# Three inputs of a linear-attention stage read head dimension first, and part of VectorE's work given to TensorE, ScalarE and GpSimd

## The reference

```
# 1. linear attention with a decaying state, per batch and head
for t in range(S):
    cur = einsum('d,e->de', u * k[t], v[t])
    y[t] = einsum('d,de->e', r[t], state + cur)
    state = w[t][:, None] * state + einsum('d,e->de', k[t], v[t])
# 2. mixture of 8 experts, top 2 by noisy gate, x = y as (3072, 384), F=1024
logits = x @ w_gate;  noisy = logits + log1p(exp(x @ w_noise)) * noise
out = sum over the two best e of weight_e * (relu(x @ w1[e]) @ w2[e])
# 3. feed forward, 2048 wide
h = out @ w_in;  result = (h - tanh(h)) @ w_out
```

## Time and profile before

| | |
|---|---|
| time, median of 3 runs | 1189.33 us (1189.25 to 1194.11) |
| the profiled execution | 1191.79 us, its span 1190.3 us |
| PE, DVE, ACT, POOL busy | 1104.0, 738.1, 567.3, 136.8 us |
| attention stage | from the start to about 227 us |
| experts, feed forward | to about 770 us, to the end |

### The profile page before, as it was taken

The page is one execution under the profiler, slowest core; times in us unless marked ns, Lnnn a source line. Parts: engine busy times, 40 slices in busy tenths (PEclk is TensorE's granted clock), DMA queues, the critical chain, the costliest instruction groups (busy, mean ns, idle before and its releaser), DMA issues.

```text
span 1190.3 us, 24896 instructions
## 1 busy us (share of the span) xinstructions
PE 1104.0 (93%) x8968; PEld 1053.2 (88%) x8968; DVE 738.1 (62%) x1036; ACT 567.3 (48%) x808; POOL 136.8 (11%) x188
## 2 busy tenths in 40 slices
PE   5888867789799999999999999999999999999998
PEld 4677756689799999999999999899999999999998
DVE  8999988638957777766677777643434333343433
ACT  5445433346347666666666666532332323333232
POOL 1000223212820000000000000221010101101010
PEclk9999889889999999999999999999999999999999
DMA  9664555556778888888888888511010101101010
GB/s 154 122 123 88 121 117 157 175 189 190 258 245 288 280 278 269 281 277 276 276 273 289 264 276 282 184 47 36 25 60 0 59 0 59 59 0 59 0 59 20
DMA packets 192751, 185.04 MB, mean 155 GB/s; under 512 B 98192, under 2 KB 160912, under 8 KB 192688
## 3 DMA queue, kind: packets, MB, share of 16 engines
q1 hardware_dynamic: 176208, 152.74, 44.8%
q0 software_dynamic: 6528, 20.06, 5.1%
q10 hardware_dynamic: 9952, 11.41, 2.8%
HBM read 156.85 MB, written 27.33 MB: 155 GB/s over the span
## 4 chain that ended last, share of the span: by engine, by line
PE 77%; DVE 13%; issue 5%; ACT 3%; SPq 1%; POOL 1%; DMA 1%; another core or an unknown queue 0%; DVEq 0%; ACTq 0%; POOLq 0%
PE ps L789 6%; PE ps L858 6%; PE ps L876 6%; PE ps L878 6%; PE ps L877 6%; PE ps L859 6%; PE ps L860 6%; PE ps L790 5%; PE ps L791 5%; PE ps L747 5%; PE ps L749 4%; PE ps L748 4%; PE ps L767 2%; PE ps L766 2%; PE ps L765 2%
## 5 line engine op out<-in xcount | busy, mean ns | idle before, releaser
L1590 DVE TENSOR_TENSOR w_lo<-w_raw,w_hi 128x1536 fp32r<-128x1536 f32 x140 | 244.3, 1755 | 93.3 <-ACT w_hi L909 88.1
L909 ACT ACTIVATE w_hi<-w_raw 128x1536 fp32r<-128x1536 f32 x140 | 206.5, 1488 | 24.8 <-ACT y_out L1101 12.3
L1590 DVE TENSOR_TENSOR gg<-ps,th 128x768 f32<-128x768 f32 x64 | 61.3, 957 | 168.3 <-ACT th L1148 168.3
L789 PE MATMUL ps<-w_hi,h_hi 128*128 128x384 f32 x440 | 151.0, 343 | 9.0 <-DVE h_lo L1674 8.3
L747 PE MATMUL ps<-xT_hi,w_hi 128*128 128x256 f32 x480 | 139.6, 291 | 10.9 <-issue 5.7
L791 PE MATMUL ps<-w_hi,h_lo 128*128 128x384 f32 x440 | 147.9, 336 | 0.0
L790 PE MATMUL ps<-w_lo,h_hi 128*128 128x384 f32 x440 | 147.9, 336 | 0.0
L1878 POOL DMA_INDIRECT yy<-yg,slot_g x54 | 54.2, 1004 | 751.3 <-DVE w_lo L1590 425.5
L749 PE MATMUL ps<-xT_hi,w_lo 128*128 128x256 f32 x480 | 137.2, 286 | 0.0
L748 PE MATMUL ps<-xT_lo,w_hi 128*128 128x256 f32 x480 | 137.1, 286 | 0.0
L876 PE MATMUL ps<-wout_hi,g_hi 128*128 128x384 f32 x384 | 130.4, 340 | 0.0
(11 more groups left out here) (266 smaller groups left out, 2088.1 us busy)
## 6 DMA issues: line engine op xcount, KB each, us to landing
w_raw<-in_moe_w SPq DMA_DIRECT2D x140, 768.0 KB
xt_in<-xg SPq DMA_DIRECT2D x20, 384.0 KB
yg<-y_out ACTq DMA_DIRECT2D x20, 384.0 KB
k_pad<-in_k SPq DMA_DIRECT2D x32, 144.0 KB, 3.9
v_nat<-in_v SPq DMA_DIRECT2D x32, 144.0 KB
out<-o_out SPq DMA_DIRECT2D x8, 576.0 KB
w_nat<-in_w SPq DMA_DIRECT2D x15, 288.0 KB, 3.3
r_pad<-in_r SPq DMA_DIRECT2D x30, 144.0 KB
```

The source lines that it names most:

```text
L789: pe.matmul(o, h_hi[:, f, cols], w2_hi[:, f, :], start=(f == 0), stop=False, skip_group_check=True)
L909: nc.scalar.activation(dst, src, ACT.Copy).then_inc(s, 1)
L1590: vec.tensor_tensor(dst, a, b, ALU.subtract).then_inc(s, 1)
```

## The change

The host hands over r, k and w transposed to head dimension first (`r_cols`, `k_cols`, `w_cols`), and v by pairs (`v_pairs`), beside the original arrays. They are loaded straight to where the scans and products read them, so `turn`, `straight`, `spread_in` and their buffers are gone. The cleared gaps between 48 and 64 partitions are now set by whole-buffer clears (`wz` by VectorE, `klin`, `rlin` by GpSimd). `wz` has two buffers. The range check is a ReLU with a sum along the row on ScalarE, once for each side of the range; VectorE only tests 8 sums to a batch. GpSimd makes `kr`. TensorE adds the bonus rows `bv` to the result in PSUM with two products with the identity, and ScalarE copies the result out (`tokens`). `betas` writes to the KV bank instead of A0.

```diff
@@ sync @@
+            def load_cols(e, dst, src, landed, n, h):
+                e.dma_start(dst[s][h * HB:h * HB + D, :], src[n // HP, 2 * (n % HP) + h]).then_inc(landed[s], 16)
 def next_w(n):
-                    sp.wait_ge(spread, n - 1)
-                    sp.wait_ge(w_squared, n - 1)
+                    sp.wait_ge(scanned, 2 * (n - 2) + 2)
+                    sp.wait_ge(w_checked, 2 * (n - 2) + 2)
 for p in range(NP):
-                next_w(p + 5)
-                next_k(p + 4)
                 next_v(p + 2)
-                next_r(p + 4)
+                next_w(p + 4)
+                next_k(p + 3)
+                next_r(p + 3)
@@ tensor @@
+            def add_bonus(p):
+                pe.wait_ge(bv_done, p + 1)
+                for h in range(2):
+                    pe.matmul(ps[:, Y0 + h, 0:Q * D], ident[:], bv[:, :, h, :], start=False, stop=True, skip_group_check=True)
 for p in range(NP):
                 scores(1, p)
                 betas(p)
-                back(p)
                 step(p, 0)
-                if p + 2 < NP:
-                    turn(1, p + 2)
                 outer(p)
                 step(p, 1)
                 intra(p)
                 if p + 1 < NP:
                     scores(0, p + 1)
+                    back(p + 1)
+                add_bonus(p)
                 inter(p)
                 step(p, 2)
-                if p + 2 < NP:
-                    turn(2, p + 2)
-                if p + 3 < NP:
-                    turn(0, p + 3)
                 step(p, 3)
@@ scalar @@
+                for side, sign in ((0, -1.0), (1, 1.0)):
+                    follow(act, w_checked, 2 * n + side)
+                    nc.scalar.activation(w_out_of[:]..., values, ACT.Relu, bias=limits[:, side:side + 1],
+                                         scale=sign, accum_out=over[:, n, side:side + 1]).then_inc(w_checked, 1)
 for p in range(NP):
-                keep_back(p)
                 step(p, 0)
-                straight(1, p + 2)
-                squares(p + 3)
+                chunk_products(p + 2)
                 step(p, 1)
-                chunk_products(p + 2)
+                check_range(p + 3)
                 step(p, 2)
-                straight(2, p + 2)
-                straight(0, p + 3)
-                spread_in(p + 4)
+                if p + 1 < NP:
+                    keep_back(p + 1)
+                tokens(p)
                 step(p, 3)
@@ vector @@
-            steps |= {(HP * c + 3, 3): [lambda c=c: finish(c)] for c in range(B - 1)}
+            steps |= {(4, 0): [lambda: finish(0)], ... (8, 0): [lambda: finish(1), lambda: softplus_2(0)], ...
+                      ... (12, 0): [lambda: finish(2), lambda: placed(1)],
 def bonus(p):
+                v_.wait_ge(KV_full, p + 1)
 for p in range(NP):
+                decayed_r(p + 1)
                 mask(1, p)
+                bonus(p)
-                bonus(p)
                 step(p, 1)
-                decayed_r(p + 1)
                 states(p)
                 step(p, 2)
                 prefix_scan(p + 2)
-                products(p + 1)
-                see(p + 3)
-                tokens(p)
                 step(p, 3)
@@ gpsimd @@
+            def products(*pairs):
+                for n in pairs:
+                    po.wait_ge(k_in_s[n % 2], 32 * (n // 2 + 1))
+                    po.wait_ge(r_in_s[n % 2], 32 * (n // 2 + 1))
+                    if n > 0:
+                        po.wait_ge(rPW_r, n + 1)
+                        po.wait_ge(KV_full, n)
+                    po.tensor_tensor(kr[:], klin[n % 2][:], rlin[n % 2][:], ALU.mult).then_inc(kr_r, 1)
```

More of the change, by code:

```diff
@@ L522, in _ @@
             pe.wait_ge(setup, 1)
-            def turn(which, n):
-                s, use = n % 2, n // 2 + 1
-                t = T_USE["wkr"[which], n]
-                if which == 0:
-                    pe.wait_ge(spread, n + 1)
-                else:
-                    pe.wait_ge((k_in_s, r_in_s)[which - 1][s], 32 * use)
-                for half in range(2):
-                    follow(pe, T_copied[half], t)
-                    for a in range(SL // 2):
-                        block = w_pad[:, 2 * a + half] if which == 0 else (k_pad, r_pad)[which - 1][s][:, half * QT + a]
-                        mm = pe.transpose(ps[:, TB[half], a * P:(a + 1) * P], block.rearrange("p h d -> p (h d)"), ident[:])
-                    mm.then_inc(T_full[half], 1)
             def scores(t, p):
@@ L684, in step @@
                     part()
-            pe.wait_ge(gaps, 1)
-            for which in range(3):
-                turn(which, 0)
-            turn(0, 1)
+            pe.wait_ge(setup, 1)
             scores(0, 0)
-            turn(1, 1)
-            turn(2, 1)
-            turn(0, 2)
+            back(0)
             for p in range(NP):
@@ L905, in _ @@
-            nc.scalar.activation(tick[:, 3:4], minus_mid[:], ACT.Copy)
-            act.wait_ge(gaps, 8)
+                load_cols(act, rlin, r_cols, r_in_s, 0, h)
+            act.wait_ge(wz_set, 6)
+            load_w(act, 1, 1)
+            act.wait_ge(zeroed, 4)
+            for h in range(2):
+                load_cols(act, rlin, r_cols, r_in_s, 1, h)
+            act.wait_ge(restarts, 5)
+            nc.scalar.activation(tick[:, 3:4], limits[:, 0:1], ACT.Relu)
             def cp(dst, src, s):
@@ L940, in w1_high, with tokens @@
+            def tokens(p):
+                b, hp = p // HP, p % HP
+                act.wait_ge(Y_full, p + 1)
+                cp(x_all[b][:, :, hp * PW:(hp + 1) * PW].rearrange("t q (h d) -> t h q d", h=2),
+                   ps[0:C, Y0:Y0 + 2, 0:Q * D].rearrange("t h (q d) -> t h q d", d=D), x_done)
             def w1_high(t, hf):
@@ L1002, in smooth, with first_high @@
                 ins.then_inc(sp_act, 1)
+            def first_high():
+                act.wait_ge(kr_r, NP)
+                for hf in range(2):
+                    w1_high(whole(0), hf)
             def kept(c, *places):
@@ L1538, in decayed_k @@
                     return
-                for half in range(2):
-                    v_.wait_ge(T_copied[half], T_USE["k", n] + 1)
+                v_.wait_ge(k_in_s[n % 2], 32 * (n // 2 + 1))
                 vec.tensor_tensor(c3(kG[n % 2][:]), c3(klin[n % 2][:]), w3(Gz[:])[:, :, 1:W1], ALU.mult).then_inc(kG_r, 1)
@@ L1545, in decayed_r @@
                     return
-                for half in range(2):
-                    v_.wait_ge(T_copied[half], T_USE["r", n] + 1)
+                v_.wait_ge(r_in_s[n % 2], 32 * (n // 2 + 1))
                 v_.wait_ge(scanned, 2 * n + 2)
+                follow(v_, Y_full, n - 1)
                 vec.tensor_tensor(c3(rPW[n % 2][:]), c3(rlin[n % 2][:]), w3(Pz[:])[:, :, 0:C], ALU.mult).then_inc(rPW_r, 1)
-            def products(n):
-                if n >= NP:
-                    return
-                vec.tensor_tensor(kr[:], klin[n % 2][:], rlin[n % 2][:], ALU.mult).then_inc(kr_r, 1)
             def mask(t, p):
@@ L1627, in _ @@
             prefix_scan(0)
-            see(0)
             decayed_k(0)
             decayed_r(0)
-            products(0)
             suffix_scan(1)
+            v_.wait_ge(setup, 1)
+            mask(0, 0)
             prefix_scan(1)
-            see(1)
-            see(2)
             for p in range(NP):
```

271 lines of the change are left out of this document (110 added, 161 removed).

## The result

The kernel after takes 1178.57 us (median of 10 runs, 1170.15 to 1183.56), the kernel before 1191.92 beside it: ratio 0.9889, 95% interval 0.9857 to 0.992, 13.4 us less. Three later comparisons of the same two kernels, on other chips, gave 0.9831 (0.9802 to 0.9861), 0.9838 (0.9812 to 0.9864) and 0.9825 (0.9798 to 0.9851), 19 to 21 us less. The forecast was 29.2 us less: the sign was right, the size was not.

What follows compares the result with a forecast made beforehand. VectorE was taken to bound the attention stage, TensorE the later parts. Terms of 7.2 + 23.4 + 1.4 - 2.8 = 29.2 us less gave 1160.1, rounded to 1160 us, against 1189.33; range 1151 to 1180.

Steps and rivals of the forecast that it cites:

- (a): From the start to the mask of pair 1: 24.3 against 31.52 us, 7.2 less, with the first scan at 5.4.
- (b): Fourteen pairs: 26.5 us off VectorE, range parts 1.7, waits -4.8, together 23.4 us less.
- (d): Collisions of GpSimd's product with VectorE: 2.8 us more, from late `outer` in some seven router pairs and 0.8 at the start.
- (c): Pair 15: masks no longer wait for betas and w_hi is ready earlier, 1.4 us less.
- rest of the program: The parts after the attention stage, expert and feed-forward: as long as before, moved earlier by what the stage gains.
- a plain pair of 8.57: A pair without router work, mask to mask: 10.46 less 1.89 us gives 8.57 where VectorE alone sets the period.
- the ReLU of 0.9: ScalarE's range-check ReLU of 768 columns: 0.9 us taken, with up to 0.3 for the row sum in the range.
- tile 0 follows `inter(15)`: At the attention stage's end, tile 0's rows are turned right behind `inter(15)`, expected near 197 us.
- the waits that were listed: VectorE waiting for ScalarE or `outer` at `finish`, `range_part`, (6, 1), (8, 2), pairs 10 and 14: 16.8 us, replacing 12.
- the bonus on TensorE: Two products of 288 columns a pair on TensorE, taken as 0.65 us for both.
- the ports cost more: Rival: every GpSimd product takes 0.9 us from VectorE instead of 0.2, 11.6 more, about 1172 us; chance 0.18.
- The slower rival: VectorE's instructions draw kr out in every pass, so GpSimd sets the loop; 1197 us at 2.5 us blocked; chance 0.06.

Runs made afterwards that it cites:

- first traces: First profiled executions of the unchanged kernel before and kernel after, not on one chip; `inter(15)` began at 226.35 and 214.77 us.
- side by side: Unchanged kernel before and kernel after traced on one chip; `inter(15)` began at 226.76 and 210.65 us, the traces 1185.2 and 1164.0 us.
- the short product: GpSimd's product cut to 48 of 768 columns from pair 1 on; against kernel before, ratio 0.9807 on the kernel after, 0.9698 with three reorderings added.
- the three orders: Kernel after with ScalarE's router pieces earlier, `outer` ahead of pieces at (p, 0), first GpSimd product behind first rPW; ratio 0.9735 to kernel before, in both sets.
- the base: Kernel after, unchanged, run again beside experiments; `inter(15)` at 209.45 us, ratio 0.9831 to the kernel before.
- three edits: Kernel after with, one each: ScalarE's router pieces earlier, `outer` ahead of pieces at (p, 0), GpSimd's product cut to 48 columns; ratios 0.9751, 0.9814, 0.9807 to kernel before.

## Why the prediction was wrong

| step | forecast | first traces | side by side |
|---|---|---|---|
| (a) start to mask of pair 1 | -7.2 | -3.9 | -4.2 |
| (b), (d) fourteen pairs | -23.4 + 2.8 = -20.6 | -7.2 | -11.3 |
| (c) pair 15 | -1.4 | -0.4 | -0.5 |
| rest of the program | 0 | -6.0 | -5.1 |
| sum | -29.2 | -17.6 | -21.2 |

**What failed** are the two terms of the fourteen pairs: the collisions with GpSimd's product (d) and the waits in (b). Side by side the pairs gained 11.3 us, not 20.6. Of the missing 9.3, 4.8 are VectorE's busy time, which fell by 20.6 instead of 28.2 - 2.8, and 4.5 its idle time, which grew by 9.3 instead of 4.8. That the whole came out no further off is luck: the rest of the program gained 5.1 to 6.0 us, for which nothing was forecast, and the range up to 1180, in which 1178.57 lies, was built from causes that did not come so (0.9 us a pair, slower ReLUs).

**What held.** What the change removes (1.89 us a pair, a plain pair of 8.57), the product of 1.7 (1.82), the ReLU of 0.9 plus a row sum (0.94 and 0.19), that tile 0 follows `inter(15)`, and the waits that were listed: each came where it was put, if not always at its size. Not so the bonus on TensorE: the forecast had 0.65 us, and it takes 1.07 by distance at full clock and up to 2.2 below it. In plain pairs this was hidden, since VectorE set the pace. Without collisions VectorE's work fell by 165.87 - 138.51 = 27.4 us, 28.2 forecast.

**(d), collisions, was mis-sized.** The term was 2.8, of it 0.8 at the start. At `inter(15)` the short product gave 5.2 us in the kernel after and 6.9 in the three orders (2.8 against their second trace); by the medians it gave 4.9 in the three orders, all executions apart from one another, and some 3 in the kernel after, inside the intervals. In VectorE's busy time it is 144.43 - 138.24 = 6.2 for the fourteen pairs (6.4 in the three orders), and 1.6 at the start. The prediction looked for Pz alone: "from 5.0 to 6.9 nothing of VectorE's has two SBUF inputs". In pairs with pieces at (p, 1), or with the flags' sum behind bv, small instructions stand just there, and each waits for the rest of the product, up to 1.5 us for 0.17 of work. The Trainium skill, "SBUF — State Buffer", section "Who interferes with whom", says both what the prediction used, that whoever starts second blocks fully, and what it left aside with "one SBUF input contends with nothing", that copies in their fast form also take the shared ports. The trace agrees in that a copy with one input was blocked (1.67 us in pair 9); whether it ran in that form it does not show. What the Trainium skill says in the "GPSIMD Engine Reference", section "Engine selection", that such a product is about half as fast there, agrees too: 1.82 against 0.93.

**(b), the waits, was mis-sized.** Idle time in the fourteen pairs grew by 9.3 us (18.1 to 27.4), not 4.8, and by 13.0 in the first traces. Waits priced at 2.85 and 2.5 were 2.59 and 5.57, later 3.1 to 3.4; bv's waits for `outer`, priced at 0.4 in one pair, came in six, up to 2.2 each: TensorE's pieces at (p, 0) stand ahead of `outer`. In the run with `outer` ahead of them those of pairs 10 and 14 (2.21 and 1.33 side by side) were gone and that of pair 13 fell from 2.06 to 0.40, while 0.88 in pair 6 stayed: the former were order, the last is not. The wait in pair 13 was on no list.

**(a) was mis-sized**: w landed so that Gz began at 6.78, 5.4 was forecast; kG lost 1.6, 0.8 had been set aside; and `range_part` waited 1.06 where nothing was set aside.

**(c)** gained 0.4 to 0.5, not 1.4: the mask of pair 15 no longer waits, as forecast (it had waited 1.49), but bv now waits 1.56 for `outer` there.

**The rival "the ports cost more"** (1172) came nearest in size, by luck: its reason, 0.9 us in every pair, is wrong. In plain pairs it is 0 to 0.45, and waits made up the other half. The slower rival's drawn-out product did not occur but at the start (2.38).

**The likeliest error in the reasoning** was to book kr's 0.85 us a pair as gain. The product's place is worth nothing that the times can tell, in either order: what VectorE sheds comes back as blocked instructions and as waits that its work had covered.

**What stays open.** Why the first comparison gained 6 to 7 us less than three others; its trace differs from the base's in pairs 1, 10, 12 and 14, among others by waits for `outer` and a few of TensorE's gaps beside the stores, but no run isolates it. And what shortens the rest: side by side the first matmul of tile 0 comes 3.75 us behind the start of `inter(15)` instead of 4.64 (in the first traces 4.17 instead of 4.33), some 3 of the other 4 us lie in the 110 us behind it, and why was not tried.

## What to carry to other kernels

Work moved off the bounding engine gains only what that engine then does not wait for: list, for every instruction that is taken away, the waits that it covered, above all where hand-placed pieces of other work stand behind a wait on the helping engine. Before GpSimd gets an elementwise product, go through everything on VectorE in the product's time, the smallest instructions first: each that comes second costs the rest of the product. Run the unchanged base again beside the experiments before sizing them, and size them by medians before single traces: here half or more of what three edits seemed to gain was the base's own.

## What the runs showed of the hardware

- On one chip TensorE lost up to 11 us in gaps that the profile gives to issue, the longest 3.98, beside GpSimd's indirect stores in bursts of twelve. The variants of the kernel after had no such gap on four others, one of them with the same bursts; the kernel before had 1.3 us of them on one of these.
- Some 6 of the 8.3 us of port collisions fell on instructions of 1 to 48 columns: one sum of a single number took 0.94 us in place of 0.14.
- Fourteen of sixteen `intra` at full clock, where the base had nine, gained nothing in all (`inter(15)` 0.3 us later): the granted clock of a stretch (0.87 and 0.90) says little about its length where TensorE is not what is waited for. In one pair of the same run half clock did cost VectorE 1.67 us.
